# Attention rounds reordered ahead of two routed expert layers, and the end of the kernel cut differently

## The reference

```python
# 1. gated linear attention, per batch and head
for t in range(S):
    state = alpha[t][:, None] * state + outer(k[t], v[t])
    y[t] = q[t] @ state
# 2. routed experts: x is y as [3072, 384]; 8 experts, width 1024
logits = (x / |x|) @ (emb / |emb|).T / tau
e = argmax(logits); gate = softmax(logits)[e]
x = gate * (relu(x @ w1[e]) @ w2[e])
# 3. dense network, width 2048
h = x @ w_in
out = where(h > 0, h, exp(min(h, 0)) - 1) @ w_out
```

## Time and profile before

| | us |
|---|---|
| median of 3 runs (901.72 to 905.69) | 904.02 |
| the profiled execution | 905.82 |
| its span, first to last instruction | 904.2 |
| PE busy in the span | 873.4 (97%) |
| DVE, ACT, POOL busy | 435.5, 321.8, 283.8 |
| mean granted clock of PE | 0.988 |

### The profile page before, as it was taken

How to read it: one execution, slowest core, us unless ns; L and a number is a source line. 1 busy time by engine, 2 the same in 40 slices (tenths; PEclk the granted TensorE clock), 3 DMA queues, 4 the chain that set the end, 5 groups by cost and what they waited for, 6 DMA issues and landing times. The chain is left out here.

```text
span 904.2 us, 16339 instructions
## 1 busy us (share of the span) xinstructions
PE 873.4 (97%) x5725; PEld 780.5 (86%) x5725; DVE 435.5 (48%) x828; ACT 321.8 (36%) x709; POOL 283.8 (31%) x279
## 2 busy tenths in 40 slices
PE   7999998889999999999999999999999999999994
PEld 5888887778898998998988999999999999999894
DVE  7889899662223223222224545445445445445442
ACT  4576665523222323222222233223223223223221
POOL 3235665355635674375617102001001001001001
PEclk9999999799999999999999999999999999999998
DMA  9977775668877878747617002002002002000000
GB/s 154 171 133 142 163 156 151 226 218 288 255 244 247 289 252 255 253 118 222 177 53 228 18 0 71 1 1 71 1 1 70 1 1 70 1 1 36 1 1 35
DMA packets 140975, 107.92 MB, mean 119 GB/s; under 512 B 103354, under 2 KB 129074, under 8 KB 140898
## 3 DMA queue, kind: packets, MB, share of 16 engines
q0 software_dynamic: 25696, 66.09, 23.0%
q1 hardware_dynamic: 115202, 40.79, 20.3%
HBM read 89.51 MB, written 17.35 MB: 118 GB/s over the span
## 5 line engine op out<-in xcount | busy, mean ns | idle before, releaser
L1427 POOL DMA_INDIRECT out<-of,idi x24 | 23.6, 983 | 370.1 <-DVE of L1513 305.4
L1247 PE MATMUL bank<-WX,hdTh 128*128 (+1 forms) x496 | 130.7, 345 | 3.0 <-DVE hdTl L1300 1.7
L1471 PE MATMUL bank<-xT_h,wi_h 128*128 128x512 f32 x288 | 114.2, 396 | 0.0
L1471 PE MATMUL bank<-xT_l,wi_h 128*128 128x512 f32 x288 | 113.6, 395 | 0.0
L1471 PE MATMUL bank<-xT_h,wi_l 128*128 128x512 f32 x288 | 113.4, 394 | 0.0
L1531 ACT ACTIVATE ee<-bank 128x512 f32<-128x512 f32 x96 | 57.3, 597 | 148.7 <-PE bank L1471 144.8
L1553 DVE TENSOR_SCALAR em<-ee 128x512 f32<-128x512 f32 x96 | 43.1, 449 | 136.6 <-ACT ee L1531 134.4
L1233 PE MATMUL bank<-WX,xdTh 128*128 (+1 forms) x372 | 99.6, 403 | 2.9 <-ACT xdTh L1273 1.4
L1534 ACT ACTIVATE g_h<-gg 128x512 fp32r<-128x512 f32 x96 | 60.6, 631 | 114.2 <-DVE gg L1558 112.5
L1171 POOL TENSOR_TENSOR WX<-raw_w,WX 128x3072 fp32r<-128x3072 f32 x14 | 95.7, 6834 | 15.4 <-DMA WX<-moe_w 11.4
L1562 DVE TENSOR_TENSOR g_l<-gg,g_h 128x512 fp32r<-128x512 f32 x96 | 69.4, 722 | 60.2 <-ACT g_h L1534 59.3
(11 more groups left out here) (215 smaller groups left out, 1444.1 us busy)
## 6 DMA issues: line engine op xcount, KB each, us to landing
WX<-moe_w POOLq DMA_DIRECT2D x14, 1536.0 KB, 10.0
raw_w<-moe_w POOLq DMA_DIRECT2D x14, 1536.0 KB, 8.1
xd<-sorted_x SPq DMA_DIRECT2D x31, 193.0 KB, 5.1
sorted_y<-yd SPq DMA_DIRECT2D x31, 192.5 KB, 4.3
xg<-sorted_y SPq DMA_DIRECT2D x6, 770.0 KB, 4.4
nat_a<-alpha SPq DMA_DIRECT2D x32, 144.0 KB, 3.4
nat_k<-k SPq DMA_DIRECT2D x32, 144.0 KB, 3.3
nat_q<-q SPq DMA_DIRECT2D x32, 144.0 KB, 4.4
```

The source lines that it names most:

```text
L1247: last = pe.matmul(y_out(t)[:, 0:DM], hdT[a][:, k * P:(k + 1) * P], WX[:, bass.ds(off + (b * WE + KD * F + k * DM), DM)], start=(k == 0 an ...
L1471: last = pe.matmul(bank[4 + i % 2][:, :], a[:, k, w], b[:, k, :], start=(k == 0 and m == 0), stop=(k == KD - 1 and m == 2))
```

## The change

The same matmuls are issued. What changes is order, engine and addressing:

- PE, DVE and ACT run the last two attention rounds (14 and 15) by lists of their own. S2 to S5 of round 14 go ahead of R, F, Qh0 and Qh1 of round 15. YN0(14) goes to bank 4 behind the Ys steps of round 15, KV(15) no longer waits for it.
- In the third batch, the R, Ng, Nk and Ns to Nr steps move from round 14 to round 13, among the Y steps. POOL issues the first three scatters at the head of round 14 and the other three at its end; the X steps follow them.
- The step X2 and the tensor `first` are gone. SP works out the rows of tiles 0 and 1 from the register of the first expert.
- The upper part of the first w1 is copied by ACT (V0, V1) instead of DVE (W2).
- PE reads a tile's position once (step K), ahead of the transposes of the tile before, and keeps it.
- The last six steps of `ladder` run on DVE after He1(1) instead of before Ye(0).
- Dense network: the copies of tiles 0 and 2 go to ACT and those of 1 and 3 to DVE (before the other way). In the last group, the three matmuls of O14 for tile 3 go between those of O15 for tile 1 and tile 2.
- SP instead of POOL waits for the output DMAs.

```diff
@@ routes and orders
         SOON = ({"S5": ("Rl", "Rx", "Dl")}, {"R": ("Rc", "Rb", "Ro"),
-                                             "S5": ("Rs", "Rn", "Rw", "Rd", "Y0", "Y1", "Y2", "Y3", "Y4", "Y5", "Y6", "Y7",
-                                                    "Rp", "Rr", "Ng", "Nk")}, {"Kh1": ("Ns", "Nt", "Nr"), "Qh1": ("Y8",)})
+                                             "S5": ("Rs", "Rn", "Rw", "Rp", "Rr", "Ng", "Nk", "Rd", "Y0", "Y1", "Y2", "Y3", "Y4",
+                                                    "Ns", "Nt", "Nr", "Y5", "Y6", "Y7")}, {"Qh1": ("Y8",)})
...
+            if n == PAIRS - 2:
+                out_ = [(x, n) for x in ("KT0", "KT1")] + [("Tk1", n + 1), ("A0", n), ("A1", n), ("YN0", n - 1), ("YN1", n - 1),
+                                                           ("KV", n), ("Tq1", n + 1)]
+                out_ += [(x, n) for x in ("Yi0", "Yi1", "Ys0", "Ys1")] + [("Tq0", n + 1)]
+            if n == PAIRS - 1:
+                out_ = [(x, n) for x in ("KT0", "KT1", "A0", "A1", "KV")] + [("YN1", n - 1)]
+                out_ += [(x, n) for x in ("Yi0", "Yi1", "Ys0", "Ys1")] + [("YN0", n - 1)]
...
             if n == PAIRS - 1:
-                out_ = [("M0", n), ("M1", n), ("W2", 0)] + sums + [("W0", 0), ("LA", n - 1), ("W1", 0),
-                                                                   ("NM", PARTIAL), ("N0", PARTIAL), ("N1", PARTIAL)]
+                out_ = [("M0", n), ("M1", n)] + sums + [("W0", 0), ("W1", 0), ("LA", n - 1),
+                                                        ("NM", PARTIAL), ("N0", PARTIAL), ("N1", PARTIAL)]
+            if n == PAIRS - 2:
+                out_ = [("M0", n)] + [(x, n + 1) for x in ("G", "Kh0", "Kh1")] + [("LA", n - 1)] + sums
+                out_ += [(x, n + 1) for x in ("R", "F", "Qh0", "Qh1")] + [("Y8", PARTIAL - 1)]
...
             if n == PAIRS - 2:
-                behind("Ln1", ("SP", PARTIAL * C))
+                behind("Ln1", *[("SP", PARTIAL * C + j) for j in range(2)])
+                behind("St5", *[("SP", PARTIAL * C + j) for j in range(2, C - 1)])
             if n == PAIRS - 1:
-                behind("Kt1", *[("SP", PARTIAL * C + j) for j in range(1, 3)])
-                behind("St5", *[("SP", PARTIAL * C + j) for j in range(3, 5)])
+                out_ = [(x, n - 1) for x in ("yT1",)] + [("Kt0", n), ("Kt1", n), ("V0", 0)] + [(f"St{i}", n) for i in range(1, C)]
+                out_ += [("Yn1", n - 1), ("Ln1", n - 1), ("V1", 0), ("SP", TT - 1), ("yT0", n)]
             if n == PAIRS:
-                behind("yT1", ("SP", PARTIAL * C + 5), ("SM", PARTIAL))
+                behind("yT1", ("Yn0", n - 2), ("Ln0", n - 2), ("SM", PARTIAL))
...
                 elif b == PARTIAL - 1 and r == 1:
-                    out_ += roots + [(f"X{i}", b) for i in range(X_STEPS)]
+                    out_ += roots
                 elif b == PARTIAL - 1 and r == 2:
-                    out_ += [("SC", b * C + j) for j in range(C)]
+                    out_[0:0] = [("SC", b * C + j) for j in range(HC)]
+                    out_ += [("SC", b * C + j) for j in range(HC, C)] + [(f"X{i}", b) for i in range(X_STEPS)]
@@ PE, attention
-                    acA.wait(pe, "Ln0", n - 1)
+                    if n < PAIRS - 1:
+                        acA.wait(pe, "Ln0", n - 1)
@@ ACT
+                if kind[0] == "V":
+                    ac.wait_ge(s_raw0[0], 16)
+                    cols = slice(i * KD * F // 2, (i + 1) * KD * F // 2)
+                    return ac.activation(parts_of(0)[0][:, cols], raw[0][:, cols], ACT.Copy)
@@ PE, experts
+            places = {}
             def position(t):
-                return pe.value_load(kth[0:1, t:t + 1], min_val=0, max_val=E - 1) if t >= EARLY else 0
+                if t not in places:
+                    k = pe.value_load(kth[0:1, t:t + 1], min_val=0, max_val=E - 1) if t >= EARLY else 0
+                    places[t] = (k, pe.snap(k % 2 * (2 * WE)) if t >= EARLY else 0)
+                    places.pop(t - 2, None)
+                return places[t]
@@ SP
-            poA.wait(sp, f"X{X_STEPS - 1}", PARTIAL - 1)
+            rows = [sp.snap(e * REGION + t * P) for t in range(EARLY)]
             for b in range(PARTIAL):
                 sp.wait_ge(s_scat[b], 16 * C)
             for t in range(EARLY):
-                load(t, sp.value_load(first[0:1, t:t + 1], min_val=0, max_val=XROWS))
+                load(t, rows[t])
@@ POOL, end; the wait goes to the end of SP's program
-            for t in range(GT):
-                po.wait_ge(s_out[t], 16 * GROUPS)
@@ PE, dense network
+                if i == K2 - 2 and n == GROUPS - 1:
+                    return [of_tile(i, t) for t in range(GT - 1)][-1]
                 if i == K2 - 1 and n == GROUPS - 1:
...
+                        if t == GT - 2:
+                            of_tile(K2 - 2, GT - 1)
+                        last = of_tile(i, t)
@@ DVE and PE, main lists
-            climb(ve, "vector", n_emb, len(ladder))
-            d(("Ye", 0), ("He0", 1), ("He1", 1), ("Ye", 1), ("Xe", 2), ("Xe", 3))
+            climb(ve, "vector", n_emb, n_tiles)
+            d(("Ye", 0), ("He0", 1), ("He1", 1))
+            climb(ve, "vector", n_tiles, len(ladder))
+            d(("Ye", 1), ("Xe", 2), ("Xe", 3))
...
-                d(("HT0", t), ("HT1", t))
+                d(("K", t + 1), ("HT0", t), ("HT1", t))
```

More of the change, by code:

```diff
@@ L412, in build @@
                     2, (f"H{last}",))
-        acE = Steps(sem("acE"), ["E0", "G0"] + [f"O{t}" for t in range(1, GT, 2)]
+        acE = Steps(sem("acE"), ["E0", "G0"] + [f"O{t}" for t in range(0, GT, 2)]
                     + [f"{x}{c}" for c in range(1, 4) for x in "EG"]
@@ L470, in yn_bank @@
         def yn_bank(n, i):
+            if n == PAIRS - 2 and not i:
+                return bank[4]
             return bank[(2 if n >= PAIRS - 2 else 3) if i else 5]
@@ L847, in step @@
                     acA.wait(ve, "Ln1", n)
+                    acA.wait(ve, "Ln0", n)
                     mine, new = LR[:, n // PPB * C:(n // PPB + 1) * C, :], LP[u][:, :, :]
@@ L1005, in step @@
                 if name == "U0":
-                    peA.wait(po, "Tq1", PAIRS - 1)
+                    peA.wait(po, "Tq0", PAIRS - 1)
                     veA.wait(po, "Qh1", PAIRS - 1)
@@ L1219, in step @@
                     i = int(name[2])
-                    k_ = position(t)
+                    k_, off = position(t)
                     upper_only, rest = name[3:] == "u", name == "M10" and t == 0
@@ L1237, in step @@
                 if name == "M2":
-                    k_ = position(t)
+                    k_, off = position(t)
                     pe.wait_ge(s_w, k_ * 2 + 2)
-                    off = half_of(k_)
                     veD.wait(pe, "He0", t)
@@ L1260, in do @@
                 for name, t in steps:
-                    if t < TILES:
+                    if t < TILES and name == "K":
+                        position(t)
+                    elif t < TILES:
                         ins = step(name, t)
@@ L1475, in emit, with of_tile @@
                 three = ((g_h, wo_h), (g_h, wo_l), (g_l, wo_h))
+                def of_tile(c, t):
+                    for m, (a, b) in enumerate(three):
+                        if m == 0:
+                            acE.wait(pe, f"G{c}", n)
+                        if m == 2:
+                            veE.wait(pe, f"L{c}", n)
+                        ins = pe.matmul(bank[t][:, 0:DM], a[c % 2][:, t * P:(t + 1) * P], b[:, c, :], start=False,
+                                        stop=(c == K2 - 1 and m == 2))
+                    return ins
+                if i == K2 - 2 and n == GROUPS - 1:
+                    return [of_tile(i, t) for t in range(GT - 1)][-1]
                 if i == K2 - 1 and n == GROUPS - 1:
-                    acE.wait(pe, f"G{i}", n)
                     for t in range(GT):
-                        for m, (a, b) in enumerate(three):
-                            if m == 2 and t == 0:
-                                veE.wait(pe, f"L{i}", n)
-                            last = pe.matmul(bank[t][:, 0:DM], a[i % 2][:, t * P:(t + 1) * P], b[:, i, :], start=False, stop=(m == 2))
+                        if t == GT - 2:
+                            of_tile(K2 - 2, GT - 1)
+                        last = of_tile(i, t)
                         if t < GT - 1:
@@ L1573, in _ @@
                 sp_tokens(sp, g)
+            for t in range(GT):
+                sp.wait_ge(s_out[t], 16 * GROUPS)
         @block.gpsimd
```

25 lines of the change are left out of this document (9 added, 16 removed).

## The result

| | before | after |
|---|---|---|
| median of 5 runs | 904.02 (901.72 to 905.69) | 896.30 (895.82 to 897.21) |
| the profiled execution | 905.82 | 895.87 |
| its span | 904.2 | 894.2 |
| mean granted clock of PE | 0.988 | 0.997 |

The ratio of the two kernels' runs is 0.9925 (95%: 0.9907 to 0.9944), which is 6.8 us (5.1 to 8.4); the medians differ by 7.7. I had predicted 4.1. The sign and the range hold.

A forecast was written before the change was run, and what follows sets the result against it. PE was taken as full from about 205 us, leaving gains in the last attention rounds, two hand-overs and the end. Attention 0 and -0.77 - 0.35 - 0.7 - 0.52 - 1.8 = -4.14 took median 904.02 to 899.9, range 895.0 to 903.5.

The forecast's parts named there:

- Attention: Rounds 14 and 15: a 1.95 us wait removed, a 2.8 us wait added; worth 0, from -1.5 to +1.5.
- the low clock from 157 to 167.5: Attention, after PE's wait for M1(14): the clock falls nearer 157 than 158, half pace until about 167.5.
- falls: Main forecast: the clock falls again in the attention, the rest pays; 899.9, own range 898 to 902, chance 0.57.
- holds: Rival: scatters miss the scan, PE waits 1.5 us, clock stays 2.4 GHz, Yn0(15) 4.1 sooner; 895.8, chance 0.28.
- the sign: POOL, round 14: the third batch's second scatter takes over 1.8 us, held up beside DVE's scan.
- V0, V1 and the register address: Cast on ACT, 1.4 us each, V0 hidden if its weights land early; register rows gain nothing.
- The ladder, -0.77: Hand-over to the experts: row steps cut in two start M2(1) at 192.2 instead of 193.00; lower bound 0.
- 0.85 of room: Ahead of XT(2): xd(2) lands at 196.4, XT(2) started at 197.25, so the ladder's gain fits.
- K, -0.35 and -0.7: Early position read removes idle time ahead of M10(3), -0.35, and M2(29), -0.7; both may be 0.
- The doubled price: Ahead of M2(29): -1.7 to -2.4 if the shorter gap also saves the 1.2 GHz stretch at 472 to 476.
- O14, -0.52: Last group: tile 0 ready three matmuls sooner, so the last output DMA moves by 0.52 us.
- The end, -1.8: POOL's 4.81 us closing DRAIN starts at its last issue and overlaps the landings: -1.8; rival of no gain, chance 0.10.

The follow-up runs named there:

- a3: Kernel after with output waits on POOL, position read in every step, row steps whole and O14 whole again; median 902.69 us, ratio to kernel before 0.9976.
- c0: Kernel after, unchanged, run and profiled again on the third chip; median 898.87 us, ratio to kernel before 0.9934.
- u1: Kernel after with the four waits for the output DMAs back on POOL instead of SP; median 898.83 us, ratio to kernel before 0.9949.
- u3: Kernel after with the last six row steps on DVE again ahead of Ye(0) and tile 1's copies; median 896.97 us, ratio to kernel before 0.9926.
- a1: Kernel after with all six scatters of the third batch ahead of M1(14) on POOL; median 903.23 us, ratio to kernel before 0.9978.
- b1: Kernel before with only S2 to S5 of round 14 moved ahead of R, F and Qh of round 15; median 907.92 us, ratio to kernel before 1.0027.
- a2: Kernel after with M1(14) ahead of the three scatters on POOL; median 900.12 us, ratio to kernel before 0.9941.
- v1: Kernel after with U0's second-expert weight loads behind the last batch's six scatters on POOL; median 901.99 us, ratio to kernel before 0.9988.
- v2: Kernel after with U0's second-expert weight loads between the last batch's norm steps and its scatters; median 906.06 us, ratio to kernel before 1.0015.
- v3: Kernel after with U0's load of the upper weights no longer waiting for xd(0) and xd(1); median 901.70 us, ratio to kernel before 0.9967.
- u2: Kernel after with the tile's position read anew in each of M10, M11 and M2, without K; median 897.49 us, ratio to kernel before 0.9934.

## Why the prediction came out as it did

**Attention: the step that failed.** I put 0 and the runs show 2.2 (a3's ratio). Between the single profiles of before and a3 it is 4.1 from KT(14) to M10(3) (57.25 and 53.16), but a3's profile is the fastest of its 12 runs, and that of before lay above the median. Two things were wrong in it.

The first is a size. I carried the low clock from 157 to 167.5, about as long as before, so that what the new order saves was spent again. In the profiles where it fell it was back at full level sooner: about 163.2 in c0 and 164 in u1 and u3, whose last low window is 162 to 164. There Yn0(15) comes at 21.0 and 22.6 after KT(14), against 25.05 before: 2.4 to 4.0 for the order with a fall included. I had taken the length of the low stretch over from the old order, and nothing in the rows said that it would be the same.

The second is the choice between "falls" and "holds", which I gave as 0.57 to 0.28. It is neither: of nine profiles of kernels whose order in round 14 is that of after, all with a wait of 2.07 to 2.10, it held in four and fell in five. Nor does the kernel before always lose it, as far as a run's mean clock can tell: in 18 of its 69 runs on the three chips this was 0.996 or 0.997, where it was 0.988 in the profiled execution, 0.995 in c0's with one short fall, and 0.997 in after's.

The profiled execution of after happened to be one where it held. I had 895.8 for that case, from 4.1 off at Yn0(15). There 5.4 came off (19.64 against 25.05), but only 4.3 of it reached M10(3) (52.94 against 57.25), and 0.4 of that is K's. That the median came so near to this rival is in part luck. Its condition, that the scatters miss the scan, wasn't met, since the second started 0.9 into it. Its 4.1 for the attention is nearly twice the 2.2 of a3. And the ratio puts the whole gain at 6.8, where the medians differ by 7.7.

The steps under it stood. The gate's reciprocal ended at 150.0 (said: 150.4), M0 started at 150.36 (151.0), the scan at 151.30 (152.0), all 0.4 to 0.7 sooner because the small DVE steps took a bit less than 0.22. The F scan still started at 156.71, where I had 156.65: what DVE was ahead went to the sum step that M1(14) held up, which I had not seen coming. The second scatter was held and ended 0.77 after the scan, as the row of before had it (0.76). Its length was 1.59, not the over 1.8 that I had named as the sign: it had started later within the scan than forecast. The sign should have been the end, not the length. M1(14) ended at 156.1 (said: 156.9) and PE waited 2.09 (said: 2.8).

What the Trainium skill states of this port (SBUF — State Buffer, "Who interferes with whom") would have let the second scatter end at 153.2. It ended at 153.81. Others that started inside a scan took 1.63 (after), 1.51 (a1), 1.38 (b1) and 2.34 (a2), where 0.96 is the usual length without one; the first three of these also ended 0.77 after their scans. The Trainium skill infers this for tensor_tensor and names no scan; for this scan the traces go against it.

**V0, V1 and the register address** cost and gave nothing, as said. V0 did wait for its weights, which landed later than the early end of the earlier trace rows that I had used:

```profile
160.83 1.48 ACT L907 ACTIVATE WX<-raw_w 128x1536 fp32r<-128x1536 f32 x1 [0.95 <-DMA raw_w<-moe_w]
```

That is 9.4 us from the issue at 151.4. PE was busy throughout 160 to 166, so it stayed hidden.

**Where the attention's gain went.** This I had not in the sum: I had asked what is late next for tile 2 alone. The norms of the last batch start only when `xd`(1) has landed, and PE met them at M10(1) (2.00 instead of 0.31). It met the rows of tile 2 at XT(2) (0.90 instead of 0). Together 2.6 of the 5.4. That the transfers are the limit is shown by v1, v2 and v3: all three free M10(1) (0.27, 0.27, 0.28), and v1 and v2 pay for it at XT(2) (3.86, 6.62), v3 at XT(0) (4.01).

**The ladder, -0.77.** In its place 0.71: DVE's `hdTl` now starts as soon as ACT's `hdTh` is there. I had found 0.85 of room in front of `xd`(2) and so kept the whole. The room was that of the old timing. With the attention 5.4 us sooner and the last scatter only 4.2 (37.52 against 41.72 after KT(14)), it was gone; u3 shows nothing left on the median, and 0.3 between two profiles in which PE was late. The lower bound of 0 that I gave, "if the landing slips", is what came.

**K, -0.35 and -0.7.** 0.37 and 0.75 by u2: right. The doubled price that I allowed for the second, a saved stretch at 1.2 GHz, stays open. The long gap came with a full clock in u2 (1.25) and a3 (1.22), and with a fall behind it in before (1.25) and b1 (1.22). In none of the nine profiles with the short gap (0.50 to 0.65) did the clock fall there. So the long gap isn't enough for a fall; whether it is needed for one, two cases of four against none of nine don't show. From M2(29) to H0 the fall is 1.6 us (6.66 against 5.06). It stands in the difference of the two profiles (10.0); how much of it stands in that of the medians (7.7) no run was made to show. The runs' own mean clocks say that the profiled execution of before, with 0.988, was one of the longest of its kernel: on the chip of c0 the four runs at 0.987 or 0.988 took 907.5 to 908.1 and those at 0.994 or more 903.2 to 905.4. b1's profile, with the same fall, was the highest of its 12 runs.

**Steady tiles.** From M10(3) to T0 it is 263.66 in before and in b1, and 263.23 to 263.26 in all the others. It isn't K, since u2 and a3 are among the short ones. These 0.4 stay open.

**O14, -0.52.** From H0 to the last issue it takes 417.60, 417.91 and 417.25 in the three profiles without this edit and 416.72 to 417.56, on the mean 417.13, in the ten with it. The difference of the means is 0.45. The spreads touch, and no run had this edit alone undone: it fits, and it isn't shown.

**The end, -1.8.** 1.94 by u1. What the Trainium skill says (VectorE: DVE Perf Modes, "The DRAIN you can't avoid"), 12 ns on all five engines, is near for ACT and PE (8 ns), DVE (17) and, in after, SP (7); SP's took 128 in before, and POOL's is 4813 ns wherever it waited for the landings first (before, u1, a3, b1).

**The sum with measured terms.** Ladder 0 to 0.4, K 0.37 + 0.75, O14 0.45 (not shown), end 1.94: 3.5 to 3.9, against 4.14 said. With a3's 2.2 that is 5.7 to 6.1. Measured by the ratios were 6.8 (5.1 to 8.4) and, in c0, 6.0 (4.3 to 7.5). So the parts add up within what the runs can tell, and the term that I had at 0 is the miss. What inside the attention part earns the 2.2, the earlier scatters, the lists of PE and ACT or the casts on ACT, no run takes apart; b1 shows only that the order of the sums alone doesn't.

## What to carry to other kernels

When a stretch with little work gets shorter, ask for each wait behind it what it waits for, a transfer above all: a step that stood free by 0.85 us is only free in the old timing, and the DMA engines don't speed up with the order. A large load that seems to wait for nothing useful may be waiting to keep out of the way of a small one; move it only with the bytes of the stretch added up. A step's time in one profile can be chance where the clock is concerned: compare it over several profiles, or over runs with the same mean clock. And let the engine with a long closing DRAIN be done first: a wait for output DMAs can stand on any engine that has nothing else to do.

## What the runs showed of the hardware

- POOL's closing DRAIN took 4813 ns in before, u1, a3 and b1, where POOL waited for the landings first. In after it ended 4.8 us after the end of the last indirect DMA's issue and was recorded as starting during the issues (7597 ns), beside the landings.
- Whether the granted clock falls in a pause of PE varies between executions of the same program (it held in after and fell in c0). With a wait of 2.1 us in round 14 it held in four profiles (1.00 in the windows behind it) and fell to 0.50 in five. A wait of 2.00 ahead of M10(1) held in after, one of 2.28 there fell in a2; 0.90 and 0.80 around XT(2) held in after, 1.12 and 0.80 fell in u2. In all waits of 3.5 us and more (b1 3.55, v1 3.86, v3 4.01, a1 6.45, v2 6.62), or within about 1 us behind them, the clock fell.
- A fall costs less at the end than in its place: 3.0 us at Yn0(15) became 0.5 at the dense network's start (u1), and 1.4 became 0.4 (c0), since PE then met less or nothing of the waits for `hd` and `xd`(2).
- PE reading a position from memory, with the register work behind it, cost 0.37 and 0.75 us where its queue had run dry, and nothing over the 263 us in which it had not (263.24 against 263.26).
- POOL and DVE hold each other up both ways. Beside a scan an indirect DMA's issue took up to 2.34 instead of 0.96 (a2); beside M1(14) the G scan took 2.38 instead of 1.74 (a2), and a sum step of 128x48 took 1.35 instead of 0.27 (after).
